# Second row buffer and moved conversions in an attention and two-MoE kernel

## The reference, cut to what matters

```python
# attention: u, v (4, 2496, 256), z (4, 2496, 64)
scores = matmul(z, z.T) / S
out = u * matmul(maximum(scores, 0) ** 2, v)          # per batch
# first MoE: rows with x @ w_skip > 0 go to one of 8 experts, others pass through
y[mask] = gate[mask] * (maximum(x[mask] @ w1[e], 0) @ w2[e]);  x = x + y
# second MoE: logits = x @ w_gate + modality_bias[modality_id], 8 experts, every row
out[mask] = gate[mask] * (maximum(x[mask] @ w1[e], 0) @ w2[e])
```

## Time and profile before

| | |
|---|---|
| median of 3 runs | 1515.71 us (1514.54 to 1515.93) |
| the profiled execution, its own time | 1515.54 us |
| its span, first to last instruction | 1514.0 us |
| TensorE busy | 1468.2 us (97%) |
| VectorE, ScalarE, GpSimd busy | 1011.9, 773.6, 401.1 us |
| mean granted TensorE clock | 0.993 of full |
| a relu, a square (mean) | 588, 624 ns |
| a high part, a low part on VectorE (mean) | 579, 786 ns |
| a V piece: ScalarE, GpSimd (mean) | 625, 1365 ns |

### The profile page before, as it was taken

How to read it: one execution, slowest core, us unless ns; L and a number is a source line. 1 busy time by engine, 2 the same in 40 slices (tenths; PEclk the granted TensorE clock), 3 DMA queues, 4 the chain that set the end, 5 groups by cost and what they waited for, 6 DMA issues and landing times.

```text
span 1514.0 us, 34658 instructions
## 1 busy us (share of the span) xinstructions
PE 1468.2 (97%) x11861; PEld 1292.1 (85%) x11861; DVE 1011.9 (67%) x2377; ACT 773.6 (51%) x1544; POOL 401.1 (26%) x379
## 2 busy tenths in 40 slices
PE   8999999999999999999899999999999999999994
PEld 7888978789888888788799999998888888888884
DVE  7989977999789998987666666665333333333331
ACT  6676767776677767665344444444333332333331
POOL 4133312334123424212322222224121221221211
PEclk9999999999999999999999999999999999999997
DMA  5311030212202020201533354323211111111110
GB/s 119 98 33 62 28 99 28 65 42 62 79 31 65 28 86 28 85 30 36 170 109 130 129 201 131 104 95 109 73 43 43 44 69 41 42 54 46 42 50 21
DMA packets 58018, 107.86 MB, mean 71 GB/s; under 512 B 18007, under 2 KB 32354, under 8 KB 57884
## 3 DMA queue, kind: packets, MB, share of 16 engines
q0 software_dynamic: 18464, 58.68, 11.1%
q1 hardware_dynamic: 39420, 47.48, 11.1%
HBM read 75.63 MB, written 32.04 MB: 71 GB/s over the span
## 4 chain that ended last, share of the span: by engine, by line
PE 81%; DVE 5%; issue 5%; DMA 4%; ACT 1%; POOL 1%; SPq 0%; POOLq 0%; ACTq 0%; DVEq 0%
PE pO L1436 23%; PE pS L1684 11%; PE pO L1696 10%; PE pS L1644 9%; PE pO L1627 9%; PE pS L1425 6%; PE pO L1698 5%; PE pM L1684 3%; DVE AH L1091 3%; DMA raw<-in_v_dram 2%; DMA token_rows<-xrow,dest 1%; PE pT L1675 1%; PE pT L1574 1%; PE pO L1445 1%; POOL token_rows L527 1%
## 5 line engine op out<-in xcount | busy, mean ns | idle before, releaser
L1093 DVE TENSOR_TENSOR AL<-A,AH 128x512 fp32r<-128x512 f32 (+1 forms) x400 | 314.4, 786 | 13.7
L1436 PE MATMUL pO<-AH,VH 64*128 64x512 f32 (+1 forms) x1520 | 306.7, 384 | 9.2 <-DVE xT L998 7.2
L1436 PE MATMUL pO<-AL,VH 64*128 64x512 f32 (+1 forms) x1520 | 305.4, 382 | 0.0
L1436 PE MATMUL pO<-AH,VL 64*128 64x512 f32 (+1 forms) x1520 | 305.1, 382 | 0.0
L709 ACT ACTIVATE R<-pS 128x512 f32<-128x512 f32 (+1 forms) x400 | 213.5, 588 | 150.4 <-PE pS L1425 134.8
L1091 DVE CAST AH<-A 128x512 fp32r<-128x512 f32 (+1 forms) x400 | 231.7, 579 | 39.8 <-ACT A L718 39.4
L718 ACT ACTIVATE A<-R 128x512 f32<-128x512 f32 (+1 forms) x400 | 229.8, 624 | 19.8 <-DVE AL L1093 19.4
L1696 PE MATMUL pO<-VL,AH 128*128 128x512 f32 x640 | 232.4, 399 | 0.0
L1351 DVE SCALAR_TENSOR_TENSOR AL<-pS,AH 128x512 fp32r<-128x512 f32 x120 | 83.0, 692 | 180.8 <-ACT AH L877 179.3
L1436 PEld LDWEIGHTS pO<-AH,VH 64*128 64x128 f32 x1520 | 154.2, 184 | 34.4 <-issue 12.6
L1698 PE MATMUL pO<-VL,AL 128*128 128x256 f32 x640 | 179.5, 280 | 0.0
(11 more groups left out here) (241 smaller groups left out, 2477.5 us busy)
## 6 DMA issues: line engine op xcount, KB each, us to landing
raw<-in_w_dram POOLq DMA_DIRECT2D x22, 1024.0 KB
A<-token_rows SPq DMA_DIRECT2D x21, 536.0 KB
uT<-in_u_dram SPq DMA_DIRECT2D x16, 512.0 KB
xin<-token_rows SPq DMA_DIRECT2D x24, 268.0 KB
raw<-in_v_dram SPq DMA_DIRECT2D x4, 1152.0 KB, 5.8
A<-in_w2t_dram POOLq DMA_DIRECT2D x8, 512.0 KB
raw<-in_v_dram SPq DMA_DIRECT2D x4, 768.0 KB, 8.1
raw<-in_z_dram SPq DMA_DIRECT2D x8, 368.0 KB
```

The source lines that it names most:

```text
L1093: v_.tensor_tensor(AL[k % NBUF][:, 0:n], A[k % NA][:, 0:n], AH[k % NBUF][:, 0:n].bitcast(F32), ALU.subtract).then_inc(al_ready, 1)
L1436: last = t_.matmul(pO[:, (KD * r + d) * QW:(KD * r + d) * QW + n], vv[rows, vo + k * D + d * P:vo + k * D + (d + 1) * P], a[k % NBUF][rows ...
```

## The change

A second row buffer: indices 1, 3, ... use a view of `xkeep` (free until the first expert), 0, 2, ... use `xrow`, each with its own count of landed rows; a buffer waits for index idx-2, and VectorE waits for idx-1 before it overwrites `dest`. `xrow_half(g, 0)` moves to p = 7, between relus and squares. ScalarE's conversions move to p = 3, 4, 5, 6, 8; the fifth Z piece moves, with its subtraction, to p = 3 of the next batch's first chunk, on GpSimd ahead of `scatter_chunk`. The first expert's four weight pieces are spread over chunks 16 and 17, at p = 3 and 6, with the subtractions tied to VectorE's pairs 4, 5 and 7, 8; the load of the second expert's weights follows in chunk 17. Behind the last chunk the transposes of index 20 are whole 128x128 ones into `pT`, the gate products come ahead of them, the copies are one each, and `prefixes(20)` comes ahead of the wait for the last copy.

The diff, with the lines that only change a name left out:

```diff
@@ -56,6 +56,8 @@
 STORED = 64
+MIDDLE = (3, 4, 5, 6, 8)
+SPLIT_AT = ((B - 1) * QC + 1, (B - 1) * QC + 2)
 ROUTE = 15
@@ -184,6 +186,7 @@
         xkeep = sb("xkeep", [P, 2, SUB, ROW])
+        chunk_rows = [xrow, xkeep[:, :, :, :].rearrange("p b s d -> p (b s) d")]
         x2a = xrow[:, 0:SUB, :]
...
@@ -276,6 +279,10 @@
+        def stored_rows(idx):
+
+            return rows_stored[idx % 2], (STORED if idx % 2 else 0) + 64 * ((idx + 1) // 2)
+
         def within(value, lo, hi):
@@ -384,7 +391,8 @@
                     if ph == 0:
-                        sp.wait_ge(rows_stored, 64 * CHUNKS)
+                        sp.wait_ge(*stored_rows(CHUNKS - 2))
+                        sp.wait_ge(*stored_rows(CHUNKS - 1))
                         full = sp.value_load(early[0:1, ph:ph + 1], min_val=0, max_val=2)
...
@@ -498,10 +506,12 @@
-                for n, (raw, wh, wl) in enumerate(weight_pieces(0)):
+                for m, p in enumerate((4, 7)):
+                    n = 2 * (g - SPLIT_AT[0]) + m
+                    raw, wh, wl = weight_pieces(0)[n]
                     wait(wh_ready, n + 1)
                     for half in range(2):
-                        wait(al_ready, 2 + KT * g + 2 * (2 * n + half + 2))
+                        wait(al_ready, 2 + KT * g + 2 * (p + half + 1))
                         w = half_piece(n, half)
...
@@ -524,8 +534,8 @@
                 for j in range(QT):
-                    g_.indirect_dma_start(xs, bass.IndirectOffsetOnAxis(dest[:, j:j + 1], 0), xrow[:, j, :], None,
-                                          bounds_check=GR * CAP - 1, oob_is_err=False).then_inc(rows_stored, 16)
+                    g_.indirect_dma_start(xs, bass.IndirectOffsetOnAxis(dest[:, j:j + 1], 0), chunk_rows[idx % 2][:, j, :], None,
+                                          bounds_check=GR * CAP - 1, oob_is_err=False).then_inc(rows_stored[idx % 2], 16)
@@ -552,6 +562,8 @@
                     times_u(g)
+                if c == 0 and b > 0:
+                    z_low(b, NG - 1)
                 if g > 1:
@@ -565,10 +577,11 @@
                     if c == QC - 1:
-                        for n in range(NG):
+                        for n in range(NG - 1):
                             z_low(b + 1, n)
-                if g == (B - 1) * QC + 1:
+                if g in SPLIT_AT:
                     split_low_first(g)
+                if g == SPLIT_AT[1]:
                     pool.wait_ge(wl_ready, WP)
@@ -659,14 +672,16 @@
                 act.wait_ge(xt_ready, 2 * idx + half)
+                if idx > 1:
+                    act.wait_ge(*stored_rows(idx - 2))
+                if idx == CHUNKS:
+                    s_.copy(chunk_rows[idx % 2][:, 2 * half:2 * half + 2, 0:D], pT[:, :].rearrange("p (t d) -> p t d", d=D)).then_inc(xrow_copied, 1)
+                    return
                 if half == 0:
                     act.wait_ge(lcols_made, idx)
-                    if idx == CHUNKS:
-                        act.wait_ge(route_step, ROUTE * idx + 1)
-                elif idx < CHUNKS:
+                else:
                     act.wait_ge(prefix_ready, idx)
-                act.wait_ge(rows_stored, 64 * idx)
-                to = xrow[:, 2 * half:2 * half + 2, 0:D].rearrange("p t (k r c) -> p r t k c", k=KD, r=2)
+                to = chunk_rows[idx % 2][:, 2 * half:2 * half + 2, 0:D].rearrange("p t (k r c) -> p r t k c", k=KD, r=2)
                 for r in range(2):
@@ -730,26 +745,29 @@
                         sums(g)
+                    if p == 7 and g > 0:
+                        xrow_half(g, 0)
                     if p == 9 and g > 0:
                         z_high(0, 2 + p // 2)
-                    if p % 2 == 1 and b < B - 1:
+                    if p in MIDDLE and b < B - 1:
+                        m = MIDDLE.index(p)
                         if c == QC - 3:
-                            if p == 1:
+                            if m == 0:
                                 act.wait_ge(pv_done, KT * QC * b + NBUF)
-                            v_high(b + 1, p // 2)
+                            v_high(b + 1, m)
                         elif c == QC - 2:
-                            v_high(b + 1, VU // 2 + p // 2)
-                        elif c == QC - 1:
-                            z_high(b + 1, p // 2)
-                    if g == (B - 1) * QC + 1 and p % 2 == 1 and p // 2 < WP:
-                        if p == 1:
+                            v_high(b + 1, VU // 2 + m)
+                        elif c == QC - 1 and p != 6:
+                            z_high(b + 1, min(m, NG - 2))
+                    if p == MIDDLE[0] and c == 0 and b > 0:
+                        z_high(b, NG - 1)
+                    if g in SPLIT_AT and p in (3, 6):
+                        if g == SPLIT_AT[0] and p == 3:
                             act.wait_ge(pv_done, KT * QC * (B - 1) + NBUF)
-                        split_high(0, 0, p // 2)
-                    if p == 6 and g > 0:
-                        xrow_half(g, 0)
+                        split_high(0, 0, 2 * (g - SPLIT_AT[0]) + (p == 6))
                     if p == 1 and g > 1:
@@ -1002,8 +1020,9 @@
             def row_meta(idx):
-                dve.wait_ge(rows_stored, 64 * idx)
-                v_.tensor_copy(xrow[:, :, TOK:TOK + 3], meta[:, ds(4 * idx, 4), :]).then_inc(meta_ready, 1)
+                if idx > 1:
+                    dve.wait_ge(*stored_rows(idx - 2))
+                v_.tensor_copy(chunk_rows[idx % 2][:, :, TOK:TOK + 3], meta[:, ds(4 * idx, 4), :]).then_inc(meta_ready, 1)
@@ -1044,13 +1063,13 @@
-                v_.tensor_copy(xrow[:, :, LOGITS:LOGITS + E], lg[:, :, 1, :])
+                v_.tensor_copy(chunk_rows[idx % 2][:, :, LOGITS:LOGITS + E], lg[:, :, 1, :])
                 dve.wait_ge(exp_done, idx)
                 step(v_.tensor_tensor(gates[:, :, :], gates[:, :, :], take[:, :, :], ALU.mult))
-                v_.tensor_tensor(xrow[:, :, GATE], gates[:, :, 0], gates[:, :, 1], ALU.add).then_inc(route_step, 1)
+                v_.tensor_tensor(chunk_rows[idx % 2][:, :, GATE], gates[:, :, 0], gates[:, :, 1], ALU.add).then_inc(route_step, 1)
@@ -1062,11 +1081,14 @@
                 dve.wait_ge(prefix_ready, idx)
-                dve.wait_ge(xrow_copied, 2 * idx + 2)
+                if idx < CHUNKS:
+                    dve.wait_ge(xrow_copied, 2 * idx + 2)
                 step(v_.tensor_tensor(rank[:, :, :], prefix[:, 0:QT, :], base[:, None, :].to_broadcast([P, QT, GR]), ALU.add))
                 step(v_.tensor_reduce(dest_f[:, :], rank[:, :, :], AX.X, ALU.add))
+                if idx > 1:
+                    dve.wait_ge(*stored_rows(idx - 1))
                 v_.tensor_tensor(dest[:, :], dest_f[:, :], invalid[:, ds(4 * idx, 4)], ALU.add).then_inc(dest_ready, 1)
...
@@ -1481,6 +1503,9 @@
                     for kd in range(KD):
+                        if idx == CHUNKS:
+                            last = t_.transpose(pT[:, (2 * i + kd) * P:(2 * i + kd + 1) * P], xT[:, kd, (2 * half + i) * P:(2 * half + i + 1) * P], ident[:, :])
+                            continue
                         for r, rows in enumerate(halves):
@@ -1490,17 +1515,23 @@
                 pe.wait_ge(base_ready, idx)
-                transpose_x(idx, 0)
+                if idx < CHUNKS:
+                    transpose_x(idx, 0)
+                else:
+                    pe.wait_ge(xrow_copied, 2 * idx)
                 for kd in range(KD):
                 last.then_inc(lcols_made, 1)
+                if idx == CHUNKS:
+                    transpose_x(idx, 0)
-                pe.wait_ge(route_step, ROUTE * idx + 1)
+                if idx < CHUNKS:
+                    pe.wait_ge(route_step, ROUTE * idx + 1)
                 transpose_x(idx, 1)
@@ -1580,8 +1611,8 @@
             keep_warm(pS[0], 6)
+            prefixes(CHUNKS)
             pe.wait_ge(xrow_copied, 2 * CHUNKS + 2)
-            prefixes(CHUNKS)
```

More of the change, by code:

```diff
@@ L227, in bass_attention_two_moe @@
         meta_ready = sem("meta_ready")
-        rows_stored = sem("rows_stored")
+        rows_stored = [sem(f"rows_stored{i}") for i in range(2)]
         final_step = sem("final_step")
@@ L417, in _ @@
                             if ph == 0:
-                                sp.wait_ge(rows_stored, 64 * (CHUNKS + 1))
+                                sp.wait_ge(*stored_rows(CHUNKS))
                             else:
@@ L517, in _ @@
             pool.wait_ge(consts_made, 3)
-            for n, semaphore in enumerate((rows_stored, PH[0].stored, PH[1].stored)):
+            for n, semaphore in enumerate((rows_stored[1], PH[0].stored, PH[1].stored)):
                 pool.dma_start(xs[GR * CAP + n * P:GR * CAP + (n + 1) * P, :], pad_row[:, :]).then_inc(semaphore, STORED)
@@ L1292, in _ @@
                     plan_second()
-                    dve.wait_ge(rows_stored, 64 * (CHUNKS + 1))
+                    dve.wait_ge(*stored_rows(CHUNKS))
                 lo = 0
```

## The result

The changed kernel takes 1497.47 us (median of 4 runs, 1496.53 to 1498.29) against 1515.82 us before (4 runs, 1514.54 to 1516.02), a ratio of 0.9881 with a 95% interval of 0.9863 to 0.9898. That is 18.3 us less. The forecast was 1502.7 us with a range of 1500.0 to 1508.0: the direction is right, the gain is larger than any case that I had written down. The profiled execution of the changed kernel took 1498.29 us (span 1496.8), 17.25 us less than that of before.

What follows compares the result with a forecast made beforehand. With TensorE busy 97% of the span, only its short gaps could be saved: 3.4 + 3.1 + 3.1 + 3.4 = 13.0 us off 1515.54 gives 1502.5, 1502.7 for the median; range 1500.0 to 1508.0.

Steps and rivals of the forecast that it cites:

- part 2: V pieces away from the edge: ScalarE's wait for V rows goes in chunks 3, 8, 13; gain 3.1 us.
- part 3: Fifth Z piece's subtraction behind the batch edge: VectorE's addition stops TensorE less in chunks 5, 10, 15; gain 3.1 us.
- part 4: First expert's weight pieces spread over chunks 16 and 17: gain 3.4 us of 3.8.
- Part 1: Second row buffer: row copies stop waiting for the scatter in chunks 5, 10, 19; gain 3.4 us.
- Part 5: Hand-over behind the last chunk: what is shortened is hidden by the first rows' load; costed at nothing.
- moved, not removed: Rival: VectorE owes the same work at the edges; part 3 gives 0, part 4 1.9, time 1507.3; chance 0.15.
- The buffer was not the cause: Rival: another wait follows the scatter waits at the same place; part 1 gives 0, time 1506.1; chance 0.05.
- the bunch of four: Rival: four V subtractions back to back hold VectorE in six V chunks; without cover, time 1533; chance 0.05.
- The hand-over's clock: Rival: low-clock stretch before the first expert, 1.7 us, goes or grows; time 1501.0 or 1504.4; chance 0.08.

Runs made afterwards that it cites:

- the old places: The changed kernel with its V and Z pieces converted at p = 1, 3, 5, 7, 9 as before: 1501.72 us, ratio 0.9911.
- the moves alone: The kernel before with V and Z conversions at p = 3, 4, 5, 6, 8 and the fifth Z piece behind the edge, one row buffer: 1509.15 us.
- the last kernel: The changed kernel without the 40 tiny keep_warm products ahead of the first expert, and 72 put into TensorE's wait for the first rows: 1492.61 us.

## Why the prediction was wrong in size

The mechanisms of parts 1 to 4 were right; the terms of the sum were too small. **The failed step** is the one that turned chunk lengths into prices: "A chunk in which nothing else happens lasts 259.33 - 224.13 = 35.20 us", with the excess of every chunk taken over it, and chunks 4, 9 and 14 not taken at all. Each part's upper bound was then that excess, so that even the largest sum, 14.7, lay below the 16.9 us that attention gave. The profile of before did hold the right yardstick for chunks 3, 8 and 13: chunk 18, which has no V or weights in it and like them stands ahead of a 448-wide chunk, lasts 686.54 - 651.64 = 34.90 us.

```profile
686.54 0.39 PE L1445 MATMUL pO<-AH,VH 64*128 64x512 f32 x2
```

Its last scores, made for the next chunk, are already 448 wide. Against it chunks 3, 8 and 13 have an excess of 1.28, 1.36 and 1.52, which is what they gave, to 0.04.

The yardstick and the chunks left out explain 1.7 of the 3.9 us by which the five terms fell short: 0.9 in chunks 3, 8 and 13, and the 0.8 of chunks 4, 9 and 14. Another 1.7 is what I held back: 0.2 in part 2, 1.1 in part 3 and 0.4 in part 4 were put as left over or rounded off, and nothing was left over. The last 0.5 is small, 0.3 of it chunk 19. Part by part:

- **Part 2 (V away from the edge)**, forecast 3.1, measured 4.14 in chunks 3, 8, 13 and 0.83 in 4, 9, 14. The mechanism was right (the load is late at p = 1: the waits of 1.17 to 1.65 us come back with the old places), the term was taken over the wrong chunk and left out the chunk behind. "Left over I put 0.2 for all three" was wrong: nothing is left over.
- **Parts 1 and 3 in chunks 5, 10, 15**, forecast 5.6, measured 6.93. "A stall of 1.28 in chunk 5 (and 10) less 1.10 leaves 0.2; in chunk 15 the stall is 1.68 and leaves 0.6" is the second failed step: no stop is left in any of the three. The 1.10 us for one subtraction was right (1.10, 1.07, 1.16 on undoing it). Two things were missed. The 1.10 was taken from a stall that had 0.17 of refill added to it, while the idle time itself was 1.11: a difference of nothing. VectorE's addition in fact starts 1.25 us earlier (2.33 instead of 3.58 us after the tail product), so a stop of 1.11 goes whole. And the 1.51 us of chunk 15 was one execution's: with the piece ahead of the edge that stop is 1.03 to 1.08 in four other kernels, 1.29 in a fifth, so that 1.10 covers it in the four.
- **The terms were added, but parts 1 and 3 are not independent.** In chunks 5 and 10 the moves alone gain 0.59 together, the buffer alone 2.69, both 5.34. With one buffer the stop in mid-chunk grows when the one at the edge goes. The sum of single gaps, read from a profile in which both stand, was right for both removed together; for the moves alone it would have been wrong by 1.6 us (2.2 from the terms of part 3 in these two chunks).
- **Part 1 in chunk 19**, forecast 0.89, measured 1.18 (1.16 with the buffer alone). **Part 4**, forecast 3.4, measured 3.81 (3.83 alone): the 0.4 held back was not needed. Here the plain chunk was the floor, and it was reached.
- **Part 5 (hand-over)**, forecast 0, measured 0.58 from the end of attention to the first expert in the full change, and no change by itself (1.0006). "What is shortened ends before 732.27 and is hidden by that load" holds as far as the issue of the load, which comes 9.8 us after attention in both, and TensorE waits for it longer, 4.62 us. But the rows are in use 0.98 us sooner after the issue, and the lower clock takes back 0.39. In the six traces that have both the buffer and the reordering, issue to use is 3.5 to 3.8 us, in the seven others 4.2 to 5.1. Why the load is quicker no run isolates; the prediction had no term for it.
- **The rest** of the 5.2 us between 1502.7 and 1497.47: 3.9 from the five terms above, 0.6 of the hand-over, less 0.4 since attention starts that much later (45.76 against 45.35); 0.9 since the profiled execution of before lay 0.28 below the median of its runs and that of after 0.8 above, of which the forecast had allowed for 0.2. That makes 5.0; 0.2 is in chunks outside the table and behind the first expert.

The low end of the range, 1500.0, failed with them. It rested on "The bounds added up give gains of 6.0 to 14.7": the range allowed for no error of the yardstick, and each term was set a few tenths low on top, so that all errors went in one direction.

Of the rivals, *moved, not removed* falls: the old cost isn't owed at another place, as chunks 16 and 17 at 35.2 and the edges without a stop show, and the changed kernel lies below 1507.3. With one buffer a like thing is true for another reason: there the cost saved at the edge of chunk 5 was owed again in mid-chunk, as a wait for the scatter. The Trainium skill, GPSIMD Engine Reference, section Key points, has GpSimd share its SBUF interfaces with VectorE; the runs agree that a subtraction at the edge holds VectorE by about 1.1 us, and that a bunch of them in mid-chunk held it for 5.68 us, at no cost to TensorE. *The buffer was not the cause* falls with the buffer alone, and *the bunch of four* with chunks 2, 7 and 12 at 35.2 us, though the bunch itself came. *The hand-over's clock* is real and its size stays within the 1.7 us given: 1.0 us between traces with the same code. The 4.9 us of the last kernel are for the larger part the 40 products, which the prediction had not looked at.

## What to carry to other kernels

Take the length of an undisturbed stretch from one with the same neighbours, not from the plainest, and let the upper bound of a gain be the time that is missing against it, chunk by chunk, those that look free included. Two stops in one chunk are not two prices: if the later one ends with a transfer, taking away the earlier feeds it, so a part must be judged with the other present and with it absent. Take an engine's delay from the idle time that it causes, not from the idle time with its refill added. Where every term of a sum is held back by a few tenths, the errors go the same way, and the range has to hold the case in which all of them are at their best.

## What the runs showed of the hardware

A scatter whose instructions are issued while the DMA engines are full lands late: the copy that needs it starts 5.3 to 6.3 us after the last instruction's end in chunk 5 of the six kernels with one buffer (DMA share 0.91 to 1.04 from 197 to 207 us), and 1.8 us after it in chunk 15 of the two in which it waits there (0.34 and 0.35). No run takes the loads away alone, so that they are the cause is argued, not shown.

The stretch at the lower clock at the hand-over differs where the code is the same from the last chunk on (granted clock 0.62 and 0.63 in two traces, 0.73 in two others, 1.0 us apart), and the runs of one kernel lie in steps: the changed kernel's are 1496.53, 1496.74 and 1498.21, 1498.29 us. The Trainium skill, TensorE: Matmul & The Clock Gate, section Part 1, says that how much work runs cold is run-variable. No profile here repeats a kernel, and a step is 1.6 us, so that the steps are the clock is argued too; that the clock can be kept full through the wait is shown by the last kernel, whose windows all read 1.00.

In mid-attention a stop of 1.1 us left the clock at 1.00, one of 2.18 us too, and one of 2.82 us was followed by 0.92 and 0.74 over 5 us each.

GpSimd's four V subtractions of a bunch held one high part on VectorE for 5.68 us, three of them 4.43.
